# Storing each attention tile's keys once, with a product of its own for the memory columns

## What is computed

```python
for c in range(nc):                       # nc = 24 chunks of 32
    q_c = q[:, :, c_start:c_end]
    k_ctx = k[:, :, l_start:r_end]        # up to 16 + 32 + 8 rows
    k_full = np.concatenate([mem_k, k_ctx], axis=2)
    scores = scale * np.matmul(q_c, k_full.transpose(0, 1, 3, 2))
    scores = scores - np.max(scores, axis=-1, keepdims=True)
    a = np.exp(scores)
    a = a / (np.sum(a, axis=-1, keepdims=True) + 1e-09)
    out[:, :, c_start:c_end] = np.matmul(a, v_full)
```

## Time and profile before

| | us |
|---|---|
| median of 3 runs | 1201.0 (1200.87 to 1211.89) |
| the profiled execution | 1206.25 |
| its span, first to last instruction | 1204.6 |
| mean granted TensorE clock | 0.950 |

### The profile page before, as it was taken

The page is one execution under the profiler, slowest core; times in us unless marked ns, Lnnn a source line. Parts: engine busy times, 40 slices in busy tenths (PEclk is TensorE's granted clock), DMA queues, the critical chain, the costliest instruction groups (busy, mean ns, idle before and its releaser), DMA issues. The chain is left out here.

```text
span 1204.6 us, 29663 instructions
## 1 busy us (share of the span) xinstructions
PE 1080.5 (90%) x7899; PEld 887.1 (74%) x7900; DVE 655.0 (54%) x1346; ACT 269.3 (22%) x520; POOL 301.6 (25%) x432
## 2 busy tenths in 40 slices
PE   5887687999999999999999999655689999999995
PEld 4766575888888888888888888544578888787774
DVE  2888686564553635535555264138286246476850
ACT  3455211221212212212212212133011212212120
POOL 1012013332322322332233233200123223232321
PEclk9989699999999999999999999877699999999997
DMA  9998945786675866757777575370387447787851
GB/s 347 352 329 311 321 159 164 229 235 182 206 221 131 244 177 183 225 145 203 211 199 211 148 201 141 77 208 12 135 271 240 143 160 235 229 251 232 294 158 32
DMA packets 123885, 245.38 MB, mean 204 GB/s; under 512 B 14367, under 2 KB 67759, under 8 KB 123857
## 3 DMA queue, kind: packets, MB, share of 16 engines
q1 hardware_dynamic: 45504, 112.25, 27.1%
q10 hardware_dynamic: 61728, 90.25, 22.7%
q0 software_dynamic: 16624, 42.54, 16.0%
HBM read 169.39 MB, written 76.39 MB: 204 GB/s over the span
## 5 line engine op out<-in xcount | busy, mean ns | idle before, releaser
L1546 PE MATMUL moe_ps_y<-weights,moe_h_hi 128*128 (+1 forms) x640 | 260.9, 408 | 15.5 <-DVE moe_h_lo L1654 15.0
L1546 PE MATMUL moe_ps_h<-weights,moe_x_hi 128*128 (+1 forms) x640 | 253.6, 396 | 22.2 <-DVE moe_x_lo L1635 21.3
L1548 PE MATMUL moe_ps_y<-weights,moe_h_lo 128*128 (+1 forms) x640 | 252.9, 395 | 0.0
L1547 PE MATMUL moe_ps_y<-weights,moe_h_hi 128*128 (+1 forms) x640 | 252.8, 395 | 0.0
L1548 PE MATMUL moe_ps_h<-weights,moe_x_lo 128*128 (+1 forms) x640 | 251.5, 393 | 0.0
L1547 PE MATMUL moe_ps_h<-weights,moe_x_hi 128*128 (+1 forms) x640 | 251.4, 393 | 0.0
L1654 DVE SCALAR_TENSOR_TENSOR moe_h_lo<-moe_h_moved,moe_h_hi 128x256 fp32r<-128x256 f32 x320 | 114.4, 420 | 240.8 <-ACT moe_h_hi L1618 240.6
L1618 ACT ACTIVATE moe_h_hi<-moe_h_moved 128x1024 fp32r<-128x1024 f32 x80 | 84.9, 1061 | 397.0 <-PE moe_ps_y L1548 344.7
L142 DVE TENSOR_TENSOR weights<-stage,weights (+1 forms) x128 | 156.8, 1225 | 20.7 <-DVE weights L140 20.4
L1546 PEld LDWEIGHTS moe_ps_h<-weights,moe_x_hi 128*128 128x128 f32 x640 | 121.6, 190 | 53.9 <-issue 24.3
L1546 PEld LDWEIGHTS moe_ps_y<-weights,moe_h_hi 128*128 128x128 f32 x640 | 122.2, 191 | 41.4 <-issue 14.7
(11 more groups left out here) (228 smaller groups left out, 780.8 us busy)
## 6 DMA issues: line engine op xcount, KB each, us to landing
stage<-in_w SPq DMA_DIRECT2D x128, 512.0 KB, 4.3
h_d<-moe_h_turned ACTq DMA_DIRECT2D x80, 512.0 KB, 3.2
moe_h_moved<-h_d ACTq DMA_DIRECT2D x320, 128.0 KB
v_sb<-in_v SPq DMA_DIRECT2D x24, 520.0 KB, 5.9
k_sb<-in_k SPq DMA_DIRECT2D x24, 512.0 KB, 6.4
x_d<-zero SPq DMA_DIRECT2D x26, 256.0 KB, 4.2
q_sb<-in_q SPq DMA_DIRECT2D x24, 256.0 KB, 4.4
x_d<-x_sb ACTq DMA_DIRECT2D x24, 256.0 KB, 5.8
```

Of the source, the lines that this page charges most:

```text
L1546: pe.matmul(out, a_hi, b_hi, start=(i == 0), stop=False)
L1547: pe.matmul(out, a_hi, b_lo, start=False, stop=False)
L1548: mm = pe.matmul(out, a_lo, b_hi, start=False, stop=(i == len(parts) - 1))
```

## The change

The key tile becomes [128, 4, 160]: KEYS = 16 + 128 + 8 = 152 context columns once, and the 8 memory columns once. A chunk's score product reads 56 columns from 32 ch on, overlapping its neighbours'. The memory columns of all four chunks come from one product a head (j and a), with all 128 queries as the stationary operand and 8 moving columns, put after each j's eight chunk products. The layout in `ps_s` stays; values, v and q stay. The last product of the last j still signals `s_done`.

```diff
+KEYS = LEFT + P + RIGHT
...
-            self.k = [sb(f"k_sb{i}", [P, HJ, NC4, WIN]) for i in range(NB)]
+            self.k = [sb(f"k_sb{i}", [P, HJ, KEYS + NM]) for i in range(NB)]
...
-                sp.dma_start(att.k[i][:, :, :, :], k[t]).then_inc(sem(f"qk_in{i}"), 16)
+                sp.dma_start(att.k[i][:, :, :], k[t]).then_inc(sem(f"qk_in{i}"), 16)
...
                     for ch in range(NC4):
                         for a in range(2):
                             part, rows = slice(a * D, (a + 1) * D), slice(ch * CHUNK, (ch + 1) * CHUNK)
-                            mm = pe.matmul(out[rows, a, j * WIN:(j + 1) * WIN], att.q[i][part, j, rows],
-                                           att.k[i][part, j, ch, :], start=True, stop=True)
+                            pe.matmul(out[rows, a, j * WIN:j * WIN + CTX], att.q[i][part, j, rows],
+                                      att.k[i][part, j, ch * CHUNK:ch * CHUNK + CTX], start=True, stop=True)
+                    for a in range(2):
+                        part = slice(a * D, (a + 1) * D)
+                        mm = pe.matmul(out[:, a, j * WIN + CTX:(j + 1) * WIN], att.q[i][part, j, :],
+                                       att.k[i][part, j, KEYS:KEYS + NM], start=True, stop=True)
                 mm.then_inc(sem("s_done"), 1)
...
+    def padded(rows, pad):
         left, right = (np.broadcast_to(pad, (B, H, n, pad.shape[-1])) for n in (LEFT, RIGHT))
...
+        return np.concatenate([left, rows, right], axis=2)
...
+    def windows(rows, starts, size, mem):
+        w = np.stack([rows[:, :, s:s + size] for s in starts], axis=2)
+        m = np.broadcast_to(mem[:, :, None], (B, H, len(starts), NM, mem.shape[-1]))
+        return np.concatenate([w, m], axis=3)
...
+    k = windows(padded(a["k"], a["mem_k"][:, :, 0:1]), range(0, S, P), KEYS, a["mem_k"])
+    k = k.reshape(B, 2, HJ, G, KEYS + NM, D).transpose(0, 3, 1, 5, 2, 4).reshape(NT, P, HJ, KEYS + NM)
```

More of the change, by code:

```diff
@@ L1841, in laid_out @@
     q = a["q"].transpose(0, 2, 1, 3).reshape(tiles).transpose(0, 1, 3, 5, 4, 2).reshape(NT, P, HJ, P)
-    def windows(rows, mem, pad):
+    def padded(rows, pad):
         left, right = (np.broadcast_to(pad, (B, H, n, pad.shape[-1])) for n in (LEFT, RIGHT))
[L1845 to L1848, removed]
+        return np.concatenate([left, rows, right], axis=2)
[3 more added lines that the diff above has]
+        return np.concatenate([w, m], axis=3)
     def with_one(rows):
         return np.concatenate([rows, np.ones_like(rows[..., :1])], axis=3)
-    k = windows(a["k"], a["mem_k"], a["mem_k"][:, :, 0:1])
-    v = windows(with_one(a["v"]), with_one(a["mem_v"]), np.zeros((B, H, 1, D + 1), np.float32))
-    k = k.transpose(0, 3, 1, 6, 2, 4, 5).reshape(NT, P, HJ, NC4, WIN)
+    k = windows(padded(a["k"], a["mem_k"][:, :, 0:1]), range(0, S, P), KEYS, a["mem_k"])
+    k = k.reshape(B, 2, HJ, G, KEYS + NM, D).transpose(0, 3, 1, 5, 2, 4).reshape(NT, P, HJ, KEYS + NM)
+    v = windows(padded(with_one(a["v"]), np.zeros((B, H, 1, D + 1), np.float32)), range(0, S, CHUNK), CTX,
+                with_one(a["mem_v"])).reshape(B, 2, HJ, G, NC4, WIN, D + 1)
     v = v.transpose(0, 3, 1, 5, 2, 4, 6).reshape(NT, P, HJ, NC4, D + 1)
```

## The result

The changed kernel takes 1253.35 us, the median of four runs (1250.07 to 1256.50). The kernel before took 1205.18 beside it (four runs). The ratio is 1.039, with an interval of 1.036 to 1.043: the change costs 48 us. The profiled execution took 1256.5 us, 50.2 more than that of before (1206.25).

A forecast was written before the change was run, and what follows sets the result against it. PE's own instruction stream, not the loads, was taken to bound the attention front. 40.7 (22 tiles) - 3.6 + 2.1 + 4.0 + 7.2 + 1.0 - 1.3 = +50.1 us on the median of 1201.0 gave 1251 us, range 1222 to 1275.

The forecast's parts named there:

- the faster rival: Rival, chance 0.03: DMA engines bound the front, so 4.7 MB less loading saves 11.6 us, giving 1189 us.
- A change of shape costs time: In each tile's scores, switching costs 0.15 us to the memory products and 0.19 us back to the chunk products.
- 1.85 us a tile: Added time from last gate matmul to first transpose at full clock, 2.83 for 0.98; range 1.53 to 2.49.
- four groups of four passes: The memory products' passes in a tile's scores, 0.20 us a group from first to last start, 0.80 in all.
- the exit: The change of shape from a tile's scores to the next transpose, taken as 0.15 us.
- eight more slow tiles: In the front, a lower granted clock slows eight more of 22 tiles by 0.9 us each: +7.2 us.
- half clock throughout: Rival, chance 0.09: the clock stays at half through the front, giving 1305 us.
- The covers: In the front, two waits of 1.3 us for probabilities and one of 1.0 for xT absorb longer scores: -3.6 us.
- The start: At the kernel's start, two key tiles 384 KB smaller, at about 300 KB a us, save 1.3 us.
- scores(23) before a wait of 4.35: At the front's end, the last scores precede a 4.35 us wait for DVE's one-hot rows, so their lengthening is covered.
- Code: Through the first loop pass, 160 more instructions, 0.6 of a block still to be fetched, cost +1.0 us.
- The wait for k1 near 2 us or less: Sign at the start: PE's wait for the second key tile, 3.16 us before, falls to near 2 us or less.

The follow-up runs named there:

- e4: Kernel before with only the smaller 320 KB key loads, its 32 products a tile kept, some memory columns left out: 1205.43 us, ratio 0.998.
- e5: Kernel before with its 512 KB loads kept, but the changed kernel's order of products: 1261.66 us, ratio 1.047.
- e3: Changed kernel with a memory product per chunk and head in the chunk products' own shape, 64*32, 32 products for 8: 1221.77 us, ratio 1.011.
- e1: Changed kernel with a tile's eight memory products put together behind all its chunk products, row halves alternating: 1239.89 us, ratio 1.030.
- e9: Kernel before with the gate product's 16 moving columns broadcast to 96, the other results unread: 1202.01 us, ratio 0.996.
- e2: As e1, but all memory products of one row half, then all of the other: 1272.1 us, a single run.
- e10: Changed kernel with the gate product's 16 moving columns broadcast to 96, the other results unread: 1253.76 us, ratio 1.038.

## Why the prediction was right, point by point

The forecast of 1251 us (1222 to 1275) met a measured 1253.35. The mechanism held: the order of PE's work makes the loss, by changes of shape and by added passes. The number is nearer than the sum deserved. Two of its large sizes were off, in opposite directions, and that they cancelled is luck.

**TensorE is the bound, the loads are not.** Right. e4 excludes the faster rival, e5 puts the loss into the order.

**A change of shape costs time, between 64*32 and 64*128 too.** Right: 0.14 us to the memory products and 0.18 back at full clock, for 0.15 and 0.19 in the sum. The price was taken from changes of other shapes, since no row had this one. e3 excludes the number of passes: four times as many without changes cost 0.56 us a tile, not 1.53. e1 takes out six of the seven changes with the same wide passes, and 0.57 us a tile go. The Trainium skill, TensorEngine Tiling (Array Packing), Key Properties, states that a change of tiling mode drains the engine; the runs agree in that a gap stands there, for two modes that differ only in columns too. What the engine does in the gap they do not show.

**1.85 us a tile.** Mis-sized. The step was "four groups of four passes (first to last start 0.12 to 0.36; I take 0.20)". Measured is 0.14, near the lower end, which agrees with the Trainium skill, TensorE: Matmul & The Clock Gate, Part 3, that weight loads overlap with running matmuls only where their row groups differ; bursts and changes were 0.01 us shorter each. First to last MATMUL is 2.14 us, and with the exit's 0.18 for 0.15 the difference is 1.53, the lower end of the range. Times 22 this is 33.7 us for 40.7.

**The clock.** Mis-sized the other way. The sum had 2.1 + 4.0 + 7.2 = 13.3 us: slower passes where the clock was low anyway, and eight more slow tiles. Measured over 19 tiles, from the first score matmul of one tile to that of the next, the mean period is 7.72 us for 5.10. At full clock it is 6.21 for 4.54. So 1.51 us a tile lie above the best tile, where it was 0.56: 0.95 more, or 18 us over the 19 tiles. Not all of the 0.56 and of the 1.51 is clock; waits and the routing between tiles are in them. By e9 only 0.10 of the 0.56 is clock. The extra cost of the lower clock is then between 0.95 us a tile, if as much waiting stands in the 1.51 as in the 0.56, and 1.4, if none does: 18 to 27 us, an estimate that the runs do not narrow further. The term that was mis-sized is the count of slow tiles: the mean clock fell from 0.90 to 0.66, where eight further tiles of 22 at 0.69 give about 0.79 (an estimate by the prediction's own figures). The rival "half clock throughout" was closer to what happened to the clock than its chance of 0.09 said, but full clock came back at times, and so 1305 was not reached.

**The covers.** Two waits of 1.3 us and one of 1.0 were to take up 3.6 us, and these three are gone. But the reading behind them was short: the gate product waited another 2.4 us for DVE's xT and 2.1 for ACT's probabilities. All waits of PE for ACT and DVE fell from 13.3 to 5.9 us, 7.4, and not 3.6. At the end I counted scores(23) as covered, 1.5 us or more, and forgot the rest of that cover: from the last row behind the scores (55.3 us late) to the first expert product (50.25 late) 5.0 us were taken back, 4.35 of them the wait before the places. The step that failed is "scores(23) before a wait of 4.35": a longer front reaches the places late by all its tiles, so the whole wait is there to be used, not one tile's part of it.

**The start.** Two key tiles were to give 1.3 us. Scores(1) begin at 8.99 for 9.43, 0.44 earlier, and 0.12 in e4 with the same loads. The rate of about 300 KB a us, taken from a stretch with other loads in flight, did not carry over to a difference of 384 KB; why, no run shows.

**Code.** One more block, as forecast (14 for 13). That it costs 1.0 us no run shows: PE's stops that nothing releases come to 5.2 us in the first 40 us before, and to 0.8 after.

The account by rows, then: 33.7 for 22 tiles at full clock; 20.5 for clock, waits and code; 0.4 less at the start; scores(23) +1.5 and the end's cover -5.0; together 50.3 for a measured 50.2. The 20.5 is what is left of the 55.3 once 23 x 1.53 and the start are taken off. It can be found again in the periods: of the 2.62 us that a tile got longer, 1.53 is the scores at full clock, 0.14 the rest of the tile at full clock (6.21 less 4.54 is 1.67), and 0.95 stands above the best tile; 19 x 1.09 is 20.7. How much of it is clock and how much waits was not measured. The prediction's near hit is made of 7 us too much in the passes and some 10 too little in the remaining terms up to there, of which the end's cover took back 3.5.

**What would have shown it wrong.** 8,283 MATMULs: so. Scores 2.5 us: 2.14. A tile 6.4 us at full clock: 6.21. The wait for k1 near 2 us or less: 0.82, though mostly because PE itself comes later, not because the keys come earlier. Scores ending near 175 us: 182. Gaps around the memory products: there.

## What to carry to other kernels

On a TensorE-bound stretch, count changes of array shape as instructions with a price, and read it from the start-to-start time in the trace; keep products of one shape together, and neighbours in different row halves. Before saving bytes in memory or on a queue, look who waits for whom: 4.7 MB less were worth nothing here, and the order they forced cost 48 us. When an edit adds short matmuls or pauses, price the granted clock as well, with the whole front at the lower level as a serious case.

## What the runs showed of the hardware

- A change between 64*32 and 64*128 holds TensorE for 0.14 us one way and 0.18 the other at full clock, though both use the same rows, and the weight load of the new shape starts only behind this gap. From the gate or to the transposes (128*128) it was 0.14 to 0.20.
- 16 passes of 64 by 128 take 0.81 us from first to last start when row halves alternate (e1), and the scores get 0.47 us longer when they do not (e2).
- The granted clock of a stretch 94% busy was 0.66; it was 0.90 at 81% and 0.98 at 77% busy with wider gate matmuls (e9). Busy share alone does not tell the clock. At full clock throughout, e9's tiles were only 0.10 us shorter than those of before.
- The clock row reads 1.00 in the first tens of us of some runs where the transposes go at 1.11 us for four, the pace of half clock; in e10 this lasts to 76 us and puts 0.79 where the pace gives some 0.64. The pace of a known group is the safer reading.
